# Attention heads leave TensorE with channels on partitions: layout prepared outside, states by one scan, outputs moved into x inside SBUF

## The reference

```python
# attention: B, H, S, D = 2, 8, 768, 48; a state of 48 x 48 per head, decayed by w at each step
for t in range(S):
    cur = einsum('bhd,bhe->bhde', u * kt, vt)
    y[t] = einsum('bhd,bhde->bhe', rt, state + cur)
    state = wt[..., None] * state + einsum('bhd,bhe->bhde', kt, vt)
x = y as (B*S, H*D) = (1536, 384)
# dense experts: P from exp(x @ w_gate) by 8 rounds of row and column scaling
out += P[:, e:e+1] * (relu(x @ w1[e]) @ w2[e])        # 8 experts, F = 1024
# routed experts: the one best expert per token, by cosine similarity
out[mask] = gate_w[mask, None] * (relu(x[mask] @ w1[e]) @ w2[e])
```

## Time and profile before

| what | us |
|---|---|
| median of three runs | 1198.9 |
| the profiled execution | 1201.32 |
| its span | 1199.6 |
| start to the first `increments` (first pair) | 24.47 |
| from there to the `increments` of the eighth pair | 113.25 |
| from there to the last write of `x_tok` | 12.6 |
| `to_channels` with its barriers | 16.1 |
| the experts | 1033.2 |

### The profile page before, as it was taken

How to read it: one execution, slowest core, us unless ns; L and a number is a source line. 1 busy time by engine, 2 the same in 40 slices (tenths; PEclk the granted TensorE clock), 3 DMA queues, 4 the chain that set the end, 5 groups by cost and what they waited for, 6 DMA issues and landing times. The chain is left out here.

```text
span 1199.6 us, 18556 instructions
## 1 busy us (share of the span) xinstructions
PE 1161.1 (97%) x6968; PEld 1039.6 (87%) x6968; DVE 504.4 (42%) x949; ACT 448.9 (37%) x926; POOL 243.8 (20%) x247
## 2 busy tenths in 40 slices
PE   6999989999999999999999999999999998999997
PEld 4888769899999998999999899999999986999997
DVE  5777556222222222212222222212222353999996
ACT  4565352212212211221221122122123473888884
POOL 5544262202201210220221121022012210000001
PEclk9888799999999999999999999999999999999999
DMA  9741043040050031005005002200300303999991
GB/s 187 144 70 31 2 149 124 26 160 1 1 186 1 1 132 55 1 2 185 1 1 185 1 1 91 94 1 1 105 1 1 132 35 114 392 358 368 359 361 59
DMA packets 106982, 123.41 MB, mean 103 GB/s; under 512 B 52745, under 2 KB 95406, under 8 KB 106912
## 3 DMA queue, kind: packets, MB, share of 16 engines
q1 hardware_dynamic: 104928, 117.65, 31.1%
q0 software_dynamic: 1984, 4.75, 1.0%
HBM read 98.37 MB, written 25.39 MB: 103 GB/s over the span
## 5 line engine op out<-in xcount | busy, mean ns | idle before, releaser
L973 DVE SCALAR_TENSOR_TENSOR h_lo<-hid,h_hi 128x512 fp32r<-128x512 f32 x168 | 116.1, 691 | 497.8 <-ACT h_hi L836 497.8
L836 ACT ACTIVATE h_hi<-hid 128x512 fp32r<-128x512 f32 x168 | 100.5, 598 | 547.7 <-PE hid L1131 547.7
L794 POOL TENSOR_TENSOR w_lo<-raw,w_hi 128x384 fp32r<-128x384 f32 x128 | 130.8, 1022 | 644.2 <-ACT w_hi L828 644.2
L1144 PE MATMUL acc<-w_hi,h_hi 128*128 128x384 f32 x736 | 249.6, 339 | 0.0
L1144 PE MATMUL acc<-w_hi,h_lo 128*128 128x384 f32 x736 | 249.3, 339 | 0.0
L1144 PE MATMUL acc<-w_lo,h_hi 128*128 128x384 f32 x736 | 248.6, 338 | 0.0
L1131 PE MATMUL hid<-x_hi,w_hi 128*128 128x512 f32 x576 | 227.9, 396 | 0.5 <-issue 0.4
L1131 PE MATMUL hid<-x_hi,w_lo 128*128 128x512 f32 x576 | 227.6, 395 | 0.0
L1131 PE MATMUL hid<-x_lo,w_hi 128*128 128x512 f32 x576 | 227.3, 395 | 0.0
L1144 PEld LDWEIGHTS acc<-w_lo,h_hi 128*128 128x128 f32 x736 | 138.1, 188 | 8.6
L1144 PEld LDWEIGHTS acc<-w_hi,h_hi 128*128 128x128 f32 x736 | 138.1, 188 | 7.7
(11 more groups left out here) (255 smaller groups left out, 1464.1 us busy)
## 6 DMA issues: line engine op xcount, KB each, us to landing
raw<-in_moe_w SPq DMA_DIRECT2D x54, 1536.0 KB, 9.2
rows<-filler SPq DMA_DIRECT2D x8, 2328.0 KB, 16.4
m_x<-rows SPq DMA_DIRECT2D x19, 194.0 KB, 4.6
spread_w<-in_w SPq DMA_DIRECT2D x16, 144.0 KB, 4.2
spread_r<-in_r SPq DMA_DIRECT2D x16, 144.0 KB, 4.1
spread_k<-in_k SPq DMA_DIRECT2D x16, 144.0 KB, 4.3
v_sb<-in_v SPq DMA_DIRECT2D x16, 144.0 KB, 4.2
out_y<-m_y,m_token POOLq DMA_INDIRECT x19, 6.7
```

Source lines behind the costliest of these rows:

```text
L794: pool.tensor_tensor(lo[q][m][:, a:b], raw[m][:, a:b], hi[q][m][:, a:b].bitcast(F32), ALU.subtract).then_inc(s_wlo, 1)
L836: act.activation(h_hi[st % HB][:, :], hid[st % HB][:, :], ACT.Relu).then_inc(s_hhi, 1)
L973: dve.scalar_tensor_tensor(h_lo[st % HB][:, :], hid[st % HB][:, :], 0.0, h_hi[st % HB][:, :].bitcast(F32), ALU.max, ALU.subtract).then_inc ...
L1144: mm = pe.matmul(acc[j][:, 0:DM], a[st % HB][:, j * P:(j + 1) * P], b[q][1][:, f * DM:(f + 1) * DM], start=(f == 0 and x == 0), stop=(f == ...
```

## The change

**Inputs.** The arrays are handed to the kernel in another layout: r, k and w already with channels on partitions (w with the zero or one that the scans need in each block's first column), v in the order in which it lies in SBUF, u as columns per pair. So `turn_in` and `channels` are gone, and six of the eight transfers of a pair write 48 rows of some 3 KB.

**The term with u.** One GpSimd product r*k (`receiver_keys`), six TensorE products with two columns of `u` (`sums`), a ScalarE copy of 12 columns (`current`); `cur_v` is transposed into the output's PSUM bank as its first contribution.

**States.** One scan over 240 elements takes the place of a copy and four steps; GpSimd lays out its factors (`carry`). The block diagonal is gone.

**Outputs.** `out_tiles` swaps its operands, so that channels come out on partitions. ScalarE copies them (`y_ch`), transfers within SBUF move them into `x_ch`, and `high_part`/`low_part` split them, half of that within the attention.

**Order.** The forward scan stands ahead of `states` on VectorE; both halves of `scores` follow one another, each with its own PSUM banks; `divided(j, 1)` stands behind the copy of the outputs; only 5 `keep_clock` products remain, at the start. `to_channels` becomes `gating`, without transposes; the buffers share the room of the experts' weights.

```diff
+FIRST, BACK, MIDDLE, LAST = 5, 0, 0, 0
...
         @block.sync
+            def load(dst, src, n, i):
+                for h in two:
+                    sp.dma_start(dst[i % 2][64 * h:64 * h + D, :], src[i, h]).then_inc(s_in[n][i % 2], 16)
+            def load_pair(i):
+                if i == 0:
+                    sp.wait_ge(s_ones, 4)
+                if i >= 2:
+                    sp.wait_ge(s_suf, i - 1)
+                load(w_pad, w, "w", i)
...
+            def put_pair(i):
+                b, j = i // (H // 2), i % (H // 2)
+                sp.wait_ge(s_ych, 2 * i + 2)
+                if b:
+                    sp.wait_ge(s_xlo, min(j + 1, KD))
+                for p, chunk, row, n in places(i):
+                    sp.dma_start(x_ch[row:row + n, chunk, :], y_ch[i % 2][p:p + n, :]).then_inc(s_x[i % 2], 16)
+            for i in range(PAIRS + 3):
+                if 4 <= i:
+                    put_pair(i - 4)
+                if i < PAIRS:
+                    load_pair(i)
+            put_pair(PAIRS - 1)
...
         @block.gpsimd
+                pool.tensor_tensor(rk[:, :], r_ch[j % 2][:, :], k_ch[j % 2][:, :], ALU.mult).then_inc(s_rk, 1)
...
+                pool.tensor_copy(carry[q][:, :, 1:NT - 1],
+                                 coef_r[:, 1:NT - 1, BT].unsqueeze(1).broadcast_to([P, D, NT - 2])).then_inc(s_carry, 1)
...
+            receiver_keys(0)
+            for j in range(PAIRS):
+                scaled(j)
+                if j + 1 < PAIRS:
+                    receiver_keys(j + 1)
+                current_values(j)
...
         @block.scalar
+            current(0)
+            for j in range(PAIRS):
+                divided(j, 0)
+                rows(j)
+                halves(j)
+                if j >= 1:
+                    outputs(j - 1, 1)
                 divided(j, 1)
+                if j + 1 < PAIRS:
+                    current(j + 1)
+                if j >= 3 and (j - 3) % (H // 2) < KD:
+                    high_part((j - 3) // (H // 2), (j - 3) % (H // 2))
+                outputs(j, 0)
+            outputs(PAIRS - 1, 1)
...
         @block.vector
-                dve.tensor_copy(st[:, 1, :], inc[:, 0, :]).then_inc(s_step, 1)
-                for t in range(1, NT - 1):
-                    dve.wait_ge(s_step, (NT - 2) * i + t)
-                    step = dve.scalar_tensor_tensor(st[:, t + 1, :], st[:, t, :], coef_r[:, t, BT:BT + 1], inc[:, t, :], ALU.mult, ALU.add)
+                dve.tensor_tensor_scan(state[q][:, :, :].rearrange("p d t -> p (d t)"), carry[q][:, :, :].rearrange("p d t -> p (d t)"),
+                                       turn[:, 0:(NT - 1) * D], 0.0, ALU.mult, ALU.add).then_inc(s_state, 1)
...
+                if ahead:
+                    before_block(i + 1)
                 if back:
                     states(i)
-                if ahead:
-                    before_block(i + 1)
...
         @block.tensor
+            def sums(j):
+                for t in range(NT):
+                    mm = pe.matmul(turn[:, CUR + 2 * t:CUR + 2 * t + 2], rk[:, t * P:(t + 1) * P], u_cols[:, j % (H // 2), :],
+                                   start=True, stop=True, skip_group_check=True)
...
                 for n in range(g * TG, (g + 1) * TG):
+                    at = slice(n % TG * P, (n % TG + 1) * P)
+                    pe.transpose(yps[g][:, at], cur_v[:, n, :, :].rearrange("p h d -> p (h d)"), ident[:, :])
+                    for h in two:
+                        if n:
+                            pe.matmul(yps[g][64 * h:64 * h + D, at], state[q][64 * h:64 * h + D, :, n - 1],
+                                      r_tile[q][64 * h:64 * h + D, n * P:(n + 1) * P], start=False, stop=False, skip_group_check=True)
+                    for h in two:
+                        mm = pe.matmul(yps[g][64 * h:64 * h + D, at], v_sb[:, i, h, n, :], scores_sb[g][h][:, n % TG, :],
+                                       start=False, stop=True, skip_group_check=True)
...
+            sums(0)
+            for j in range(PAIRS):
+                pe.wait_ge(s_cur, j + 1)
+                keep_clock(FIRST if j == 0 else BACK)
+                turn_back(j)
+                if j >= 1:
+                    out_tiles(j - 1, 1)
+                increments(j)
+                scores(j, 0)
+                scores(j, 1)
+                keep_clock(MIDDLE)
+                if j + 1 < PAIRS:
+                    sums(j + 1)
+                out_tiles(j, 0)
+            keep_clock(LAST)
+            out_tiles(PAIRS - 1, 1)
...
 gating, on ScalarE (before: nine x_hi and sixteen pieces of w_hi in turn, then three gate_rows)
+            for c in range(len(PIECES)):
+                if c in (2, 5):
+                    chunk = 1 + c // 5
+                    for q in range(2):
+                        act.wait_ge(s_x[q], moved(q, H // 2 + chunk + 2))
+                    act.activation(x_hi[:, chunk, S:N], x_ch[:, chunk, :], ACT.Copy).then_inc(s_xhi, 1)
+                piece(c)
+                if c == 9 or c >= len(PIECES) - 2:
+                    g = 0 if c == 9 else c - len(PIECES) + 3
+                    act.wait_ge(s_lrow, g + 1)
```

More of the change, by code:

```diff
@@ L2 @@
+import math
 from contextlib import ExitStack
@@ L41, with places, moved, attention @@
 HEADS = ((0, 64), (64, P))
-def attention(nc, r, k, v, w, u, x_tok, ident, upper, prefetch):
+FIRST, BACK, MIDDLE, LAST = 5, 0, 0, 0
+def places(i):
+    found = []
+    for h in range(2):
+        at = (i % (H // 2) * 2 + h) * D
+        cut = min(D, P - at % P)
+        for o, n in ((0, cut), (cut, D - cut)):
+            if n:
+                found.append((64 * h + o, (at + o) // P, (at + o) % P, n))
+    return found
+def moved(q, pairs):
+    return 16 * sum(len(places(i)) for i in range(q, pairs, 2))
+def attention(nc, r, k, v, w, u, x_hi, x_lo, x_ch, s_x, s_xhi, s_xlo, spare, ident, upper, prefetch):
     G = 2
     TG = NT // G
-    FIRST, MIDDLE, LAST = 5, 2, 4
     BLK1, BT1 = BLK + 1, BT + 1
+    WP = NB * BLK1 + 1
     with ExitStack() as ctx:
@@ L62, in attention, with placed @@
         two = range(2)
[L63 to L68, removed]
+        def placed(area, shapes):
+            at = spare[area]
+            for name, shape, dt in shapes:
+                t = nc.alloc_sbuf_tensor_at(name, shape, dt, offset=at)
+                at += (4 * math.prod(shape[1:]) + 31) // 32 * 32
+                yield t
@@ L95, in attention @@
[L95 to L99, removed]
+        state = [sb(f"state{q}", [P, D, NT - 1]) for q in two]
+        carry = [sb(f"carry{q}", [P, D, NT - 1]) for q in two]
+        rk = sb("rk", [P, S])
+        cur = [sb(f"cur{q}", [P, NT, 2]) for q in two]
+        cur_v = sb("cur_v", [P, NT, 2, 64])
+        turn = ps("turn", [P, 1024])
@@ new lines, in outputs, with high_part @@
+            def outputs(i, g):
+                act.wait_ge(s_y, 2 * i + g + 1)
+                if i >= 2 and g == 0:
+                    act.wait_ge(s_x[i % 2], moved(i % 2, i - 1))
+                act.activation(y_ch[i % 2][:, g * TG * P:(g + 1) * TG * P], yps[g][:, 0:TG * P], ACT.Copy).then_inc(s_ych, 1)
+            def high_part(b, c):
+                for q in two:
+                    act.wait_ge(s_x[q], moved(q, b * (H // 2) + c + 2))
+                act.activation(x_hi[:, c, b * S:(b + 1) * S], x_ch[:, c, :], ACT.Copy).then_inc(s_xhi, 1)
@@ L602, in _ @@
-            gating(1)
-            gating(2)
             for t in range(TT):
```

457 lines of the change are left out of this document (193 added, 264 removed).

## The result

The changed kernel took **1210.1 us** in the median (1203.9 to 1216.3, 12 runs), the one before 1204.4 in the same comparison: a ratio of 1.0082, 95% interval [1.0058, 1.0106].

The account below looks back on a forecast made before the run. It took a loop over ScalarE and TensorE to bound the changed kernel's pairs. Periods -11.1, start -5.4, end 0, gating -3.5 sum to -20.0: 1201.3 becomes 1181.3, median forecast 1179 us, range 1162 to 1197.

Parts of the forecast that it names:

- Start, first increments at 19.1: Before the first pair's increments: earlier divisions and shorter `keys` were to save 5.4 us from 24.5.
- The clock share: Seven pair periods: TensorE at the low clock for 40% of the time, as measured before, making the period 14.6 us.
- third rival: Every pair: clock stays low without idle products and transposes; period 17.7 us, total 1208; chance 0.10.
- The price of a low period, 17.7: One pair period with TensorE low all the time, summed over ScalarE and TensorE: 17.7 us with hand-overs.
- ring over ScalarE: Pair period: loop from `k_rows` through ScalarE and TensorE back to `k_rows`, 12.85 us at the high clock before hand-overs.
- VectorE's ring: Pair period: loop from `k_rows` through VectorE's masks, backward scan and `keys` to the second output half, 12.3 us.
- The high period, 13.0: One pair period at the high clock, over ScalarE and TensorE: 13.0 us with six hand-overs.
- Output tile, 0.8: TensorE's new output tile at the high clock: 0.8 us, the two heads overlapping in part, no drain between tiling modes.
- second rival: Output tiles: no overlap of heads, tile 1.2 us, high period 14.0, total 1189; chance 0.15.
- Last pair, no change: End of attention: 12.0 us against 12.6 + 0.1, taken as 0, with -0.7 to +5 allowed.
- Gating, 12.6: Gating stage: ScalarE loses nine `x_hi` pieces and gains two; 12.6 us, a saving of 3.5.
- The fourth: Rival: moves inside SBUF hold up SP, loads come late; some 1.5 us in five periods, 1187; chance 0.07.

Follow-up runs that it names:

- e6: Changed kernel plus 18 full-array transposes per pair whose result nobody reads: 12 ahead of the second scores, 6 ahead of `turn_back`; 1193.8 us.
- e4: Changed kernel with 4 idle products ahead of `turn_back`, 4 behind the second scores and 4 ahead of the last output half; 1206.3 us.
- e10: Changed kernel with `sums` moved between the two halves of the scores, no idle products in the pairs; 1212.1 us.
- e12: e9 with 1 instead of 2 idle products ahead of `turn_back`; 1175.4 us.
- e7: e10 with idle products: 2 between the score halves, 2 ahead of `turn_back`, 4 ahead of the last output half; 1186.2 us.
- e9: e7 with each output half regrouped: three transposes, then all state products, then all v products; part of the sum left out; 1176.5 us.
- e11: e9 with 5 instead of 9 pieces of `w_lo` on GpSimd in the gating stage, the others on VectorE; 1175.6 us.
- e5: Changed kernel with `sums` cut from six products to one for every pair but the first; 1195.2 us.
- e8: e7 with 4 idle products between the score halves and 3 ahead of `turn_back`, instead of 2 and 2; 1196.5 us.
- e13: e12 with e11's edit, only the first transpose of an output half starting a sum, nothing left out of the sum; 1172.9 us.

## Why the prediction was wrong, step by step

- **Start, first increments at 19.1:** 19.47. Right.
- **The clock share: the step that failed.** The prediction took over the low clock's share of the time from the kernel before: "With reasons both ways I keep the measured 40%". It became 78%, a granted clock of 0.61 instead of 0.80. With my own prices, 13.0 and 17.7, that share gives 1 / (0.22/13.0 + 0.78/17.7) = 16.4 us where I had 14.6. The reasons for and against were not of equal weight. I counted waits, as if TensorE's clock followed its waits; what had gone were 18 full-array transposes and three full-array idle products per pair, and e6 and e4 show that such work alone brings the clock back, while the low periods (86.07 to 124.81, e10) have no wait at all. The earlier trace rows held the pattern: full where transposes and idle products stand close, low across the scores. I wrote it under the third rival and gave it 0.10. With the measured prices of a period, 12.8 and 19.4, a share of 40% would have given 14.8, close to the forecast.
- **The price of a low period, 17.7:** 19.37. It is the smaller error. I closed the ring over ScalarE: 0.2 + 0.5 + 2.55 + 0.8 behind the first output half, 4.05. But TensorE's own path from there, `turn_back` and the second half, is 5.9 at the low clock and outlasts it. I had followed that path for the high clock only, in VectorE's ring (12.3 beside ScalarE's 12.85). TensorE's terms at my own low prices add up to 1.2 + 2.85 + 2.85 + 2.6 + 3.9 + 1.3 + 4.6 = 19.3, and I never formed that sum. With 12.8 and 19.37 the share of 78% gives 17.4 of the measured 17.6; the last 0.2 I can't place.
- **The high period, 13.0:** 12.8, by TensorE's 12.1 and the wait of 0.7 for the divisions. Right in size, though from two errors, and so in part by luck: the output tile was 1.01 and not 0.8 (1.60 low, both over my limit of 1.0), and the ring was another. `k_rows` was done before TensorE came to it (it waited for it ahead of the first pair's increments only). The second output half's end releases its copy on ScalarE (70.80), behind which stand the divisions and then the second scores (73.88).
- **Output tile, 0.8:** the second rival's mechanism was real and smaller than its 1.2: some 0.14 per mode change (e12 against e7). My 0.8 had two errors. The heads overlap entirely (in e12 eight state records take 0.61 and twelve 0.83, so four take 0.22, a tile 0.55), and the three changes add the other 0.46. I had excluded such a pause by an average, 20 records of scores in under 0.6. But those records start in fours, 0.007 apart within a four, and the single starts in the kernel before show what the average hid: 0.087 from one four of 64x64 to the next, and 0.148 to the first of 64x32 (78.098 to 78.246). In the low period it hardly counts, 4.19 and 4.60 for the two halves where my tile gives 3.9 and 4.6; it was worth 1.2 us per period once the clock held (e7 to e9).
- **Last pair, no change:** 13.28 against 12.62, within what I allowed. **Gating, 12.6:** 14.21. I priced the stage by ScalarE and left `w_lo` out. With fewer `x_lo` pieces ahead of it, VectorE now makes its `w_lo` pieces while GpSimd makes the others, and they slow each other: a piece takes 1.36 on VectorE beside GpSimd's and 0.54 after them, in the kernel before as well. e11 brought the stage to 12.7.
- **The third rival** is what came: its 1208 by a period of 17.7 in every pair, measured 17.6 on average by longer ones in some. Its condition, slower once the period exceeds 16.4, held, though its other terms did not come (end +5, measured +0.7; gating -1.6, measured -1.9). That its total lies so near 1210 is partly luck. **The fourth** did not: no engine waited for a transfer. The experts changed by 1.4 us.

What stays open: which part of a pair's work let the clock fall. e5 excludes `sums` as the sole cause; the runs don't separate scores from output tiles. The profiled execution is 6 us below the median of its kernel; that the other runs had still more low stretches, as e10's profile has, is argued from it and not shown.

## What to carry to other kernels

Before taking "useless" full-array work out of TensorE's stream, look at the granted clock beside it: if that work stands where the clock returns, the low periods must be priced with TensorE's whole order of work, and the forecast made for a falling clock first. A few idle products can pay for themselves and more do not, so number and place have to be measured. Products on parts of the array are best grouped by tiling mode. An average over records that start in groups can't show a pause between the groups: read the single starts.

## What the runs showed of the hardware

- Adding 18 transposes per pair made the kernel 1.3% faster (e6); TensorE busy in 100% of 130.8 us had a granted clock of 0.54 (e10), and busy in 100% of 110.5 us one of 0.94 (e8).
- At the full clock a change of tiling mode between transposes (128x128), products on 48x48 and products on 128x48 cost some 0.14 us (e12 against e7).
- A 128x384 subtraction took 0.54 on VectorE once GpSimd was done with its own, and 1.36 beside them (e11). On GpSimd it took 1.02 beside VectorE's subtractions out of PSUM (before) and 1.33 beside VectorE's `w_lo` pieces, out of SBUF (e11).
- The place where a sum starts counts for a whole PSUM bank: with three transposes in one bank that each start a sum, two tiles lose `cur_v` to the later products (e9); where only the first starts one, the later transposes write without adding to what stood there, and nothing is lost (e13).
